# Reordering the start, the softmax exponentials and the last group's y in an attention, RWKV channel mix and gated convolution kernel

## The chip, the cores and the metric

One core of one Trainium2 chip. The metric is the device time of one execution in microseconds (us), the median of the runs. TensorE, VectorE, ScalarE, GpSimd and SyncE are PE, DVE, ACT, POOL and SP in the rows.

## What is computed

```python
w = np.exp(weight_gen - max); w = w / (sum(w) + 1e-9)       # softmax over 7 taps, 8 heads
x = causal 7-tap sum of x with weights w                      # attention, (2, 4160, 192)
xk, xr = mix of x and the token before it, with mu_k, mu_r
v = np.maximum(xk @ w_k, 0) ** 2 @ w_v                        # 192 -> 1024 -> 192
y = sigmoid(xr @ w_r) * v
h = np.maximum(y @ w_in, 0)                                   # 192 -> 1024
c = 3-tap convolution of h over the tokens, per channel
out = (h * sigmoid(c)) @ w_out                                # 1024 -> 192
```

## The kernel before

Each partition holds 65 consecutive tokens. They are worked through in 18 groups of 2, 2, 3, then fourteen times 4, and at last 2 token slots (a slot is 128 columns in the products); NG is the number of groups and NC = 8 the number of 128-wide chunks of the inner dimension. The order on each engine is written out by hand and kept by semaphores. In every group i the engines pass through two phases:

- `phase_a(i)`: PE makes the eight chunks of the first up product of group i+1 (`up1`, five matmuls each into one of the two PSUM banks `up0`, `up1`), the r product (`r_unit`), the transposes of y of group i (`yt_part`), and the down product of window i-1 (`down2`). ACT makes relu and square of each chunk (tile `ksq`), the high part of y, and the r sigmoid (tile `y`). DVE makes the low parts of y (`y_lo_part`), two convolution steps, the softmax of a later stretch of weights in two halves (`softmax_front`, `softmax_back`), and between the halves `attention(i+2)`.
- `phase_b(i)`: PE makes the second up product (`up2`), the down product of group i+1 (`down1`) and the transposes of attention (`t_part`). ACT makes the relu into `h` (`h_relu`), the first tap (`first_tap`), the gate's sigmoid (`gate_sigmoid`), and the copies `xt_copy` and `x_hi`. DVE makes the other taps and the gate (`window_step`), the mixes (`prep_k`, `prep_2`, `prep_r`), the low parts (`x_lo`), and y itself (`y_mult`).

A chunk of an up product may start when ACT has read the chunk two before it from the same bank. A `down1` or `down2` block is one token slot, eight matmuls of 128x192 (each stands as two in the trace).

`exps(n)` on ACT takes the exponential of stretch n of the attention weights. Exponential and sigmoid are in different activation tables; relu, square and copy need no load beside either. Stretch 0 is at the start, stretch 1 in `phase_b(0)`, stretches 2, 3 and 4 in `phase_a` of groups 2, 3 and 5.

At the very end the convolution wraps: the first two slots of `h` of group 0 are wanted again by the last window, so POOL copies them aside into `h3[:, :, KEEP + P:KEEP + 3 * P]`.

The start is a chain: the weights `wgt` arrive by three DMAs from ACT's queue, DVE makes the softmax of stretch 0, copies the parameters `prm` (which five DMAs bring, and PE transposes), then makes `attention(0)`, whose end lets PE start.

The end is written out too: `y_mult(NG - 1)`, `yt_part(NG - 1)`, `y_hi_part` and `y_lo_part` of the last group lie between the chunks of `up2(NG - 2)`, and `up2(NG - 1, 0)` needs what they make. The last group's parts use the tiles `xk_hi`, `xk_lo` and `xk2_s` (in rows `xk_s`).

Of the kernel before, what the change touches and what calls it, by code (L numbers as in the profile page):

```python
# [11 lines left out]
P = 128  # L12


def mixer_kernel(nc, x, weight_gen, mu_k, mu_r, w_k, w_v, w_r, w_in, conv_w, w_out, out):
# [58 lines left out]
    with ctx:  # L74
# [17 lines left out]
        prm = sb("prm", [P, NPRM])  # L92
        omu = sb("omu", [P, 3])

        wgt = sb("wgt", [P, (TPP + 1) * WROW])
# [56 lines left out]
        tap_act, tap, cv_ok, gs_ok, g_ok = [sem(n) for n in ("tap_act", "tap", "cv_ok", "gs_ok", "g_ok")]  # L152
        o_done, o_ok = sem("o_done"), sem("o_ok")
        h_keep, h_wrap, wrap_fix = [sem(n) for n in ("h_keep", "h_wrap", "wrap_fix")]
# [65 lines left out]
        def _(sp):  # L220
# [9 lines left out]

            S0 = size(0)
            sp.dma_start(xin[:, TAPS * D:(TAPS + S0) * D], x_rows[:, 0:S0 * D]).then_inc(x_in, 16)
            for a, b in HALO_RUNS:
# [38 lines left out]
        def _(pool):  # L272
# [20 lines left out]
            for g in range(3):  # L293
                double(g)

            pool.wait_ge(h_ok, NC)
            nc.gpsimd.tensor_copy(h3[:, :, KEEP + P:KEEP + 3 * P], h3[:, :, 0:2 * P]).then_inc(h_keep, 1)
            pool.wait_ge(h_keep, 1)
            double(3)
# [8 lines left out]
        def _(pe):  # L308
# [157 lines left out]
            for c in range(NC):  # L466
# [3 lines left out]
                if c == 5:  # L470
                    pe.wait_ge(wr_in, 32)
                    pe.wait_ge(wr_zero, 1)
                    r_unit(0, 0)
            pe.wait_ge(wv_in, 16)
            t_part(1, 1)
            t_part(1, 2)
            down1(0, 0)
            down1(0, 1)
# [17 lines left out]
            for c in range(NC):  # L496
                up2(NG - 2, c)
                if 1 <= c <= size(NG - 1):
                    down1(NG - 1, c - 1)
                if c == 4:  # L500
                    down2(NG - 3, 0)
                if c in (5, 6):
                    yt_part(NG - 1, c - 4)
                if c == 7:
                    down2(NG - 3, 1)
            for c in range(NC):
# [14 lines left out]
        def _(act):  # L521
# [52 lines left out]
            def h_relu(g, c):  # L574
                act.wait_ge(u2_done, NC * g + c + 1)
                if not eq(g, 0) and not eq(g, 1):
                    act.wait_ge(h_free, NC * n_windows(g - 1) + c + 1)
                at, n = h_home(g), size(g) * P
                nc.scalar.activation(h3[:, c, at:at + n], up[c % 2][:, 0:n], ACT.Relu).then_inc(h_ok, 1)  # L579

# [20 lines left out]
            def phase_a(i, with_y=True, with_out=True, with_o_copy=True, softmax_part=None, relus=0):  # L601

                for c in range(NC):
                    if c >= relus:
                        k_relu(i + 1, c)
                    if c >= 1:
                        k_square(i + 1, c - 1)
                    if with_y and c in (0, 2):
                        y_hi_part(i, c // 2 + 1)
                    if with_out and c in (0, 2):  # L610
                        gate_sigmoid(i - 1, EARLY + c // 2)
                    if c in (4, 6) and (c - 4) // 2 < len(units(i + 1)):
                        r_sigmoid(i + 1, (c - 4) // 2)
                k_square(i + 1, NC - 1)
                if softmax_part is not None:
                    exps(softmax_part)
                if with_out and with_o_copy:
                    for u in range(len(units(i - 1))):
                        o_copy(i - 1, u)

            def phase_b(i, with_t=True, with_win=True, softmax_part=None):
                for c in range(NC):
# [5 lines left out]
                    for part in t_parts_after(i, c) if with_t else ():  # L628
                        xt_copy(i + 2, part)
                    for part in t_parts_after(i, c - 2) if with_t else ():  # L630
                        x_hi(i + 2, part)
                    if c == 4 and softmax_part is not None:
                        exps(softmax_part)

# [5 lines left out]

            act.dma_start(wgt[:, WROW:SM_ENDS[1] * WROW], wg_rows[:, 0:(SM_ENDS[1] - 1) * WROW]).then_inc(wg_in, 16)
            for a, b in ((1, 16), (16, P)):
                act.dma_start(wgt[a:b, 0:WROW], before(wg_flat, a, b, 1, WROW)).then_inc(wg_in, 16)
            exps(0)
            act.wait_ge(wk_in, 48)
            nc.scalar.activation(wk_hi[:, :], raw_w(0), ACT.Copy).then_inc(w_cast, 1)
# [55 lines left out]
            for c in range(NC):  # L702
                h_relu(NG - 2, c)
                first_tap(NG - 2, c)
                if c >= 1:
                    gate_sigmoid(NG - 2, c - 1)
                if c in (6, 7):
                    y_hi_part(NG - 1, c - 5)
            gate_sigmoid(NG - 2, NC - 1)
# [23 lines left out]
        def _(dve):  # L733
# [247 lines left out]
            prep_r(2)  # L981
            x_lo(2, 1)
            y_mult(1, 0)
            x_lo(2, 2)
            softmax_back(1)
# [22 lines left out]
            for s in range(NC + 1):  # L1008
                window_step(NG - 2, s)
                if s == 3:  # L1010
                    y_mult(NG - 1, 0)
                if s in (6, 7):
                    y_lo_part(NG - 1, s - 5)
            for s in range(NC + 1):
                window_step(NG - 1, s)


            dve.wait_ge(h_free, NC * n_windows(NG))
            nc.vector.tensor_copy(h3[:, :, 2 * P:3 * P - 1], h3[:, :, KEEP + P + 1:KEEP + 2 * P]).then_inc(h_wrap, 1)
            nc.vector.tensor_copy(h3[:, :, KEEP + 1:KEEP + P], h3[:, :, P:2 * P - 1]).then_inc(h_wrap, 1)  # L1020
# [29 lines left out]
```

## Time and profile before

| | |
|---|---|
| time, median of 3 runs | 770.17 us (769.21 to 771.2) |
| profiled execution | 767.42 us, of which the span is 765.6 us |
| PE busy | 727.1 us, 95% of the span |
| DVE busy | 623.6 us, 81% |
| ACT busy | 485.5 us, 63% |
| POOL busy | 95.5 us, 12% |
| mean granted clock of PE | 0.995 of full speed |

The times on the left of the rows below are microseconds from the start of the span. The profiled execution was 2.75 us under the median of the other runs.

### The profile page before, as it was taken

The numbers are of one execution on the slowest core, as the hardware profiler recorded it, in microseconds if no ns is written. First come the engines' busy times: TensorE is split into PE (matmuls) and PEld (weight loads), VectorE is DVE, ScalarE is ACT, GpSimd is POOL, SyncE is SP. The second block draws the span as 40 slices with busy tenths as digits, with TensorE's granted clock in tenths as the row PEclk, the third lists the DMA queues.
The fourth block names the chain that finished last, engine by engine and source line by source line (L and its number), as shares of the span: only waits on it lengthen the run. The fifth ranks groups of instructions, "written<-read, shape, count | busy, mean of one in ns | idle before, by whom it ended". The sixth has DMA issues, their size and how long they took to land.

```text
span 765.6 us, 11918 instructions
## 1 busy us (share of the span) xinstructions
PE 727.1 (95%) x4043; PEld 664.8 (87%) x4043; DVE 623.6 (81%) x960; ACT 485.5 (63%) x913; POOL 95.5 (12%) x164
## 2 busy tenths in 40 slices
PE   0798989999999999999999999999999999999988
PEld 0697879998989899998989899898989999898988
DVE  5898899999699969869696988969696996937685
ACT  2557667676676747666674756667574765667764
POOL 1000101111110101101020111102010110101120
PEclk9999999999999999999999999999999999999999
DMA  7600110020202001020201002020200101000001
GB/s 180 212 2 0 52 63 1 0 68 1 73 1 73 0 25 49 0 72 0 72 0 61 11 0 72 0 72 0 72 0 12 60 0 62 1 22 0 1 9 55
DMA packets 8804, 27.82 MB, mean 36 GB/s; under 512 B 1007, under 2 KB 4041, under 8 KB 8647
## 3 DMA queue, kind: packets, MB, share of 16 engines
q1 hardware_dynamic: 8472, 27.21, 11.0%
q8 instruction: 17, 0.28, 0.1%
q10 hardware_dynamic: 302, 0.23, 0.1%
q14 instruction: 13, 0.10, 0.0%
HBM read 21.05 MB, written 6.39 MB: 36 GB/s over the span
## 4 chain that ended last, share of the span: by engine, by line
PE 87%; DVE 7%; ACT 4%; issue 1%; DMA 1%; ACTq 0%; DVEq 0%
PE up L346 37%; PE od L407 21%; PE dn L407 21%; PE mid L311 3%; PE dn L399 3%; PE dn L398 3%; DVE cv L855 1%; DVE prod L760 1%; DVE att L765 1%; DVE cv L857 1%; DMA wgt<-in_weight_gen 1%; ACT ksq L559 1%; ACT ksq L564 1%; DVE gat L865 1%; ACT L638 0%
## 5 line engine op out<-in xcount | busy, mean ns | idle before, releaser
L407 PE MATMUL dn<-wv_sb,ksq 128*128 128x192 f32 x1040 | 180.2, 327 | 0.7 <-ACT y L571 0.7
L407 PEld LDWEIGHTS dn<-wv_sb,ksq 128*128 128x128 f32 x1040 | 172.7, 191 | 5.7 <-ACT y L571 0.9
L855 DVE SCALAR_TENSOR_TENSOR cv<-h,prm,cv 128x512 f32<-128x512 f32 (+2 forms) x144 | 100.4, 697 | 89.5 <-ACT cv L586 88.8
L407 PE MATMUL od<-wo_sb,gat 128*128 128x192 f32 x944 | 160.9, 326 | 0.0
L407 PEld LDWEIGHTS od<-wo_sb,gat 128*128 128x128 f32 x944 | 155.3, 190 | 2.4
L559 ACT ACTIVATE ksq<-up 128x512 f32<-128x512 f32 (+2 forms) x144 | 80.0, 556 | 97.1 <-PE up L346 96.5
L291 POOL COPY h<-h 128x256 f32<-128x256 f32 x136 | 82.8, 609 | 428.0 <-DVE gat L865 396.6
L579 ACT ACTIVATE h<-up 128x512 f32<-128x512 f32 (+2 forms) x144 | 79.0, 550 | 88.9 <-PE up L346 88.8
L857 DVE SCALAR_TENSOR_TENSOR cv<-h,prm,cv 128x512 f32<-128x512 f32 (+2 forms) x144 | 101.2, 702 | 5.1
L586 ACT ACTIVATE cv<-h,prm 128x512 f32<-128x512 f32 (+2 forms) x144 | 97.9, 681 | 8.8 <-DVE h L1023 2.2
L765 DVE TENSOR_TENSOR att<-att,prod 128x768 f32<-128x768 f32 (+2 forms) x108 | 95.4, 883 | 1.6 <-DVE att L765 0.5
L760 DVE TENSOR_TENSOR prod<-xin,wgt 128x768 f32<-128x768 f32 (+2 forms) x108 | 96.0, 903 | 0.1
L591 ACT ACTIVATE cv<-cv 128x512 f32<-128x512 f32 (+2 forms) x144 | 83.6, 581 | 17.3 <-DVE cv L857 16.4
L865 DVE TENSOR_TENSOR gat<-h,cv 128x512 f32<-128x512 f32 (+2 forms) x128 | 82.3, 643 | 0.8
L564 ACT ACTIVATE ksq<-ksq 128x512 f32<-128x512 f32 (+2 forms) x144 | 82.9, 588 | 0.0
L346 PE MATMUL up<-xk_hi,wk_hi 128*128 128x512 f32 (+2 forms) x144 | 65.2, 452 | 4.2 <-ACT ksq L559 1.9
L346 PE MATMUL up<-y_hi,wi_hi 128*128 128x512 f32 (+2 forms) x136 | 63.5, 467 | 3.3 <-ACT h L579 3.2
L346 PE MATMUL up<-xk_hi,wk_lo 128*128 128x512 f32 (+2 forms) x144 | 54.7, 380 | 0.0
L346 PE MATMUL up<-xk_lo,wk_hi 128*128 128x512 f32 (+2 forms) x144 | 54.7, 380 | 0.0
L346 PE MATMUL up<-xk_s,wk_hi 128*128 128x512 f32 (+2 forms) x144 | 54.5, 378 | 0.2 <-DVE xk_s L828 0.2
L346 PE MATMUL up<-xk_s,wk_lo 128*128 128x512 f32 (+2 forms) x144 | 54.1, 376 | 0.0
L346 PE MATMUL up<-y_s,wi_hi 128*128 128x512 f32 (+2 forms) x136 | 51.7, 380 | 0.3 <-DVE y_s L848 0.3
(101 smaller groups left out, 978.5 us busy)
## 6 DMA issues: line engine op xcount, KB each, us to landing
xin<-in_x SPq DMA_DIRECT2D x13, 960.0 KB, 4.9
out<-o_sb SPq DMA_DIRECT2D x14, 384.0 KB, 2.3
wgt<-in_weight_gen SPq DMA_DIRECT2D x1, 1288.0 KB, 6.0
xin<-in_x SPq DMA_DIRECT2D x1, 864.0 KB, 4.7
wv_sb<-in_moe_w_v SPq DMA_DIRECT2D x1, 768.0 KB, 4.7
wo_sb<-in_moe_w_out SPq DMA_DIRECT2D x1, 768.0 KB, 7.8
xin<-in_x SPq DMA_DIRECT2D x1, 768.0 KB, 4.4
gat<-in_moe_w_k SPq DMA_DIRECT2D x1, 512.0 KB, 5.6
```

The costliest lines, as they stand in the source:

```text
L291: nc.gpsimd.tensor_copy(h3[:, c, 0:2 * P], h3[:, c, n:n + 2 * P]).then_inc(h_free, 1)
L346: mm = nc.tensor.matmul(dst[:, 0:n], w[:, cols], a[:, 0:n], start=(t == 0), stop=(t == len(terms) - 1))
L407: mm = nc.tensor.matmul(dst[:, n * D:(n + 1) * D], lhs(c)[:, b * P:(b + 1) * P], w[:, c, :], start=(c == 0), stop=(c == NC - 1))
L559: nc.scalar.activation(ksq3[:, c, 0:n], up[c % 2][:, 0:n], ACT.Relu).then_inc(k_ok, 1)
L564: nc.scalar.activation(ksq3[:, c, 0:n], ksq3[:, c, 0:n], ACT.Square).then_inc(ksq_ok, 1)
L586: nc.scalar.activation(conv_tile(w, c), win(w, c, 0), ACT.Copy, scale=prm[:, 3 + NC + c:4 + NC + c])\
L591: nc.scalar.activation(conv_tile(w, c), conv_tile(w, c), ACT.Sigmoid).then_inc(gs_ok, 1)
L760: nc.vector.tensor_tensor(v, x_tap(k), w_tap(k), ALU.mult)\
L765: nc.vector.tensor_tensor(acc, acc, term(k), ALU.add)\
L855: nc.vector.scalar_tensor_tensor(o, win(w, c, -1), taps[0], o, ALU.mult, ALU.add).then_inc(tap, 1)
L857: nc.vector.scalar_tensor_tensor(o, win(w, c, 1), taps[2], o, ALU.mult, ALU.add).then_inc(cv_ok, 1)
L865: nc.vector.tensor_tensor(gate_tile(w, c), win(w, c, 0), conv_tile(w, c), ALU.mult).then_inc(g_ok, 1)
```

## The change

It has six parts. (1) The main load of the first weights goes to SP's queue, ahead of x; ACT's queue keeps the two small ones, the larger of them first. (2) After the first exponential ACT makes a sigmoid of one column (tile `early`), and `down1(0, 0)` goes ahead of the transposes of group 1 on PE. (3) In `phase_b(0)` the exponential of stretch 1 moves from after the high parts of x to ahead of them, one chunk of `h` sooner, and the second x low part goes ahead of `y_mult(1, 0)` on DVE. (4) In `phase_a` the exponentials of stretches 2 to 4 move from behind the last square to behind the second r sigmoid, two squares and a relu sooner. (5) POOL's copy of the first slots of `h` goes; ACT writes each relu of group 0 twice instead, the kept one first. (6) The last group's `y_mult` is one step sooner on DVE, its transposes, high and low parts one chunk sooner, and two `down2` blocks of window NG - 3 later.

```diff
             S0 = size(0)
+            sp.dma_start(wgt[:, WROW:SM_ENDS[1] * WROW], wg_rows[:, 0:(SM_ENDS[1] - 1) * WROW]).then_inc(wg_in, 16)
             sp.dma_start(xin[:, TAPS * D:(TAPS + S0) * D], x_rows[:, 0:S0 * D]).then_inc(x_in, 16)
...
-            pool.wait_ge(h_ok, NC)
-            nc.gpsimd.tensor_copy(h3[:, :, KEEP + P:KEEP + 3 * P], h3[:, :, 0:2 * P]).then_inc(h_keep, 1)
-            pool.wait_ge(h_keep, 1)
             double(3)
...
             pe.wait_ge(wv_in, 16)
+            down1(0, 0)
             t_part(1, 1)
             t_part(1, 2)
-            down1(0, 0)
             down1(0, 1)
...
-                if c == 4:
-                    down2(NG - 3, 0)
-                if c in (5, 6):
-                    yt_part(NG - 1, c - 4)
-                if c == 7:
-                    down2(NG - 3, 1)
+                if c in (4, 5):
+                    yt_part(NG - 1, c - 3)
+                if c in (6, 7):
+                    down2(NG - 3, c - 6)
...
+                if eq(g, 0):
+
+                    nc.scalar.activation(h3[:, c, KEEP + P:KEEP + P + n], up[c % 2][:, 0:n], ACT.Relu)\
+                      .then_inc(h_keep, 1)
                 nc.scalar.activation(h3[:, c, at:at + n], up[c % 2][:, 0:n], ACT.Relu).then_inc(h_ok, 1)
...
                     if c in (4, 6) and (c - 4) // 2 < len(units(i + 1)):
                         r_sigmoid(i + 1, (c - 4) // 2)
+                    if c == 6 and softmax_part is not None:
+                        exps(softmax_part)
                 k_square(i + 1, NC - 1)
-                if softmax_part is not None:
-                    exps(softmax_part)
...
-                    for part in t_parts_after(i, c - 2) if with_t else ():
+                    if c == 3 and softmax_part is not None:
+                        exps(softmax_part)
+                    for part in t_parts_after(i, c - (1 if eq(i, 0) else 2)) if with_t else ():
                         x_hi(i + 2, part)
-                    if c == 4 and softmax_part is not None:
-                        exps(softmax_part)
...
-            act.dma_start(wgt[:, WROW:SM_ENDS[1] * WROW], wg_rows[:, 0:(SM_ENDS[1] - 1) * WROW]).then_inc(wg_in, 16)
-            for a, b in ((1, 16), (16, P)):
+            for a, b in ((16, P), (1, 16)):
                 act.dma_start(wgt[a:b, 0:WROW], before(wg_flat, a, b, 1, WROW)).then_inc(wg_in, 16)
             exps(0)
+
+            act.wait_ge(id_ok, 2)
+            nc.scalar.activation(early[:, :], ident[:, 0:1], ACT.Sigmoid).then_inc(early_ok, 1)
...
-                if c in (6, 7):
-                    y_hi_part(NG - 1, c - 5)
+                if c in (5, 6):
+                    y_hi_part(NG - 1, c - 4)
...
             x_lo(2, 1)
+            x_lo(2, 2)
             y_mult(1, 0)
-            x_lo(2, 2)
             softmax_back(1)
...
-                if s == 3:
+                if s == 2:
                     y_mult(NG - 1, 0)
-                if s in (6, 7):
-                    y_lo_part(NG - 1, s - 5)
+                if s in (5, 6):
+                    y_lo_part(NG - 1, s - 4)
...
+            dve.wait_ge(h_keep, NC)
```

On ACT in `phase_b(0)`, before, from the last squares of the phase ahead (`ksq`) through the relus (`h`), the x copies, the table load and exponential of stretch 1 (`wgt`):

```order
50 L564 ACTIVATE ksq<-ksq 128x256 x2
51 L579 ACTIVATE h<-up 128x256 x3
52 L528 ACTIVATE xt<-mid 128x384 x2
53 L579 ACTIVATE h<-up 128x256 x2
54 L536 ACTIVATE xk_hi<-xk 128x384
55 L539 ACTIVATE xk_s<-xkr 64x384
56 L638 ACT_TABLE_LOAD
57 L638 ACTIVATE wgt<-wgt 128x672
58 L579 ACTIVATE h<-up 128x256 x3
59 L559 ACTIVATE ksq<-up 128x384
```

The same place now, from the two x copies on; L577 is the kept relu and L579 the ordinary one:

```order
57 L524 ACTIVATE xt<-mid 128x384 x2
58 L577 ACTIVATE h<-up 128x256
59 L579 ACTIVATE h<-up 128x256
60 L638 ACT_TABLE_LOAD
61 L638 ACTIVATE wgt<-wgt 128x672
62 L532 ACTIVATE xk_hi<-xk 128x384
63 L535 ACTIVATE xk_s<-xkr 64x384
64 L577 ACTIVATE h<-up 128x256
65 L579 ACTIVATE h<-up 128x256
```

The exponential stands behind the fourth relu of the group instead of the fifth, ahead of both x high parts, and every relu is there twice.

On ACT in `phase_a(2)`, before, from the second r sigmoid (`y`) to the first relu of the next phase (`h`):

```order
123 L571 ACTIVATE y<-dn 128x384
124 L559 ACTIVATE ksq<-up 128x512
125 L564 ACTIVATE ksq<-ksq 128x512 x2
126 L638 ACT_TABLE_LOAD
127 L638 ACTIVATE wgt<-wgt 128x672
128 L598 ACTIVATE o_sb<-od 128x384
129 L579 ACTIVATE h<-up 128x384
```

The same place now:

```order
136 L567 ACTIVATE y<-dn 128x384
137 L638 ACT_TABLE_LOAD
138 L638 ACTIVATE wgt<-wgt 128x672
139 L555 ACTIVATE ksq<-up 128x512
140 L560 ACTIVATE ksq<-ksq 128x512 x2
141 L598 ACTIVATE o_sb<-od 128x384
142 L579 ACTIVATE h<-up 128x384
```

Table load and exponential went ahead of the last relu and the last two squares; nothing else moved.

On DVE near the end, before, from the gate of chunk 5 (into `xin`) of window NG - 2; `xk_lo` and `xk_s` are the last group's low parts of y:

```order
510 L865 TENSOR_TENSOR xin<-h,cv 128x512
511 L845 TENSOR_TENSOR xk_lo<-mid,xk_hi 128x256
512 L855 SCALAR_TENSOR_TENSOR cv<-h,prm,cv 128x512
513 L857 SCALAR_TENSOR_TENSOR cv<-h,prm,cv 128x512
514 L865 TENSOR_TENSOR prod<-h,cv 128x512
515 L848 TENSOR_TENSOR xk_s<-mid,xk_s 64x256
516 L865 TENSOR_TENSOR prod<-h,cv 128x512
```

The same place now, from the gate of chunk 4:

```order
507 L867 TENSOR_TENSOR xin<-h,cv 128x512
508 L847 TENSOR_TENSOR xk_lo<-mid,xk_hi 128x256
509 L857 SCALAR_TENSOR_TENSOR cv<-h,prm,cv 128x512
510 L859 SCALAR_TENSOR_TENSOR cv<-h,prm,cv 128x512
511 L867 TENSOR_TENSOR xin<-h,cv 128x512
512 L850 TENSOR_TENSOR xk_s<-mid,xk_s 64x256
513 L857 SCALAR_TENSOR_TENSOR cv<-h,prm,cv 128x512
514 L859 SCALAR_TENSOR_TENSOR cv<-h,prm,cv 128x512
515 L867 TENSOR_TENSOR prod<-h,cv 128x512 x2
```

Both low parts are one convolution step sooner; the last convolution (two rows into `cv`) now has both ahead of it, where it had one.

## Rows read from the trace of the kernel before

**Rows 1.** The page, shares of the chain that ended last.

```profile
PE 87%; DVE 7%; ACT 4%; issue 1%; DMA 1%; ACTq 0%; DVEq 0%
```

**Rows 2.** Who waited for whom, PE: us in total, times, longest.

```profile
PE mid L311 <- DVE att L765: 12.0, 2, 10.6
```

**Rows 3.** The chain in order of time, its first DMA: start, us, what.

```profile
1.92 4.93 DMA wgt<-in_weight_gen
```

**Rows 4.** Timeline of the first 13 us: start, us, engine, line; idle before and releaser.

```profile
4.18 0.30 SPq L239 DMA_DIRECT2D prm_rows<-in_moe_conv_w  x1
...
6.87 0.62 DVE L930 TENSOR_REDUCE smx<-wgt 128x64 f32<-128x448 f32 x1 [5.94 <-DMA wgt<-in_weight_gen]
...
9.53 0.27 PE L461 MATMUL mid<-ident,prm_rows 27*128 27x27 f32 x1 [9.53 <-DMA prm_rows<-in_moe_conv_w]
...
10.99 0.18 DVE L956 COPY prm<-mid 128x27 f32<-128x27 f32 x1
...
12.02 1.06 ACT L646 ACTIVATE wk_hi<-gat 128x1024 fp32r<-128x1024 f32 x1 [3.26 <-DMA gat<-in_moe_w_k]
```

**Rows 5.** Timeline around the first r sigmoid.

```profile
32.73 1.28 ACT L571 ACT_TABLE_LOAD   x1
...
34.57 5.47 PE L407 MATMUL dn<-wv_sb,ksq 128*128 128x192 f32 x32 [0.70 <-ACT y L571]
...
35.80 1.29 DVE L947 TENSOR_TENSOR wi_lo<-gat,wi_hi 128x512 fp32r<-128x512 f32 x2 [2.77 <-ACT wi_hi L659]
...
37.01 0.35 DVE L797 TENSOR_SCALAR xk<-xt,omu 128x256 f32<-128x256 f32 x1
```

**Rows 6.** Timeline of phase_b(0), and the exponentials by source line (ns min/median/max).

```profile
57.48 0.39 ACT L579 ACTIVATE h<-up 128x256 f32<-128x256 f32 x1 [2.81 <-PE up L346]
...
58.70 1.28 ACT L638 ACT_TABLE_LOAD   x1
...
61.09 0.39 PE L346 MATMUL up<-y_hi,wi_hi 128*128 128x256 f32 x1 [2.31 <-ACT h L579]
...
L638 ACT ACTIVATE wgt<-wgt x5: 576/768/1048, 8.2 to 238.3; 128x672 f32<-128x672 f32 x2, 128x448 f32<-128x448 f32 x1, 128x896 f32<-128x896 f32 x1, 128x1008 f32<-128x1008 f32 x1
```

**Rows 7.** Three windows: length, busy PE, PEld, DVE, ACT, POOL; granted clock, DMA, GB/s.

```profile
63.00:64.00 1.00, 1.00 (x6) 0.90 (x5) 1.00 (x1) 0.13 (x1) 1.00 (x1) 0.50 0.00 0
114.00:115.00 1.00, 1.00 (x5) 1.00 (x4) 0.96 (x3) 0.98 (x2) 0.00 (x0) 0.50 0.04 11
236.00:246.00 10.00, 10.00 (x59) 9.28 (x58) 9.20 (x12) 8.38 (x12) 0.40 (x1) 1.00 0.38 128
```

**Rows 8.** Timeline where phase_a(2) passes into phase_b(2).

```profile
111.49 0.66 PE L311 MATMUL mid<-ident,att 128*128 128x128 f32 x4 [1.39 <-DVE att L765]
...
112.84 0.69 PE L346 MATMUL up<-y_hi,wi_hi 128*128 128x384 f32 x1 [0.69 <-ACT h L579]
```

**Rows 9.** Timeline, y of group 3 and its transposes.

```profile
130.25 0.55 DVE L837 TENSOR_TENSOR y<-dn,y 128x384 f32<-128x384 f32 x1
...
131.74 0.60 PE L311 MATMUL mid<-ident,y 128*128 128x128 f32 x4
```

**Rows 10.** Timeline, the softmax after stretch 3 and y of group 4.

```profile
152.78 1.09 DVE L938 TENSOR_REDUCE smx<-wgt 128x128 f32<-128x896 f32 x1 [1.37 <-ACT wgt L638]
...
174.45 0.66 PE L311 MATMUL mid<-ident,y 128*128 128x128 f32 x4 [1.34 <-DVE y L837]
```

**Rows 11.** Timeline of the last group's y.

```profile
721.58 0.56 DVE L837 TENSOR_TENSOR y<-dn,y 128x384 f32<-128x384 f32 x1
...
730.47 0.63 ACT L591 ACTIVATE cv<-cv 128x512 f32<-128x512 f32 x1 [1.36 <-DVE cv L857]
...
731.07 0.43 DVE L848 TENSOR_TENSOR xk_s<-mid,xk_s 64x256 fp32r<-64x256 f32 x1
...
731.64 0.36 PE L346 MATMUL up<-xk_s,wi_hi 128*128 128x256 f32 x1 [2.23 <-DVE xk_s L848]
...
732.15 0.38 ACT L579 ACTIVATE h<-up 128x256 f32<-128x256 f32 x1 [1.05 <-PE up L346]
```

More of the change, by code:

```diff
@@ L93, in mixer_kernel @@
         omu = sb("omu", [P, 3])
+        early = sb("early", [P, 1])
         wgt = sb("wgt", [P, (TPP + 1) * WROW])
@@ L152, in mixer_kernel @@
         tap_act, tap, cv_ok, gs_ok, g_ok = [sem(n) for n in ("tap_act", "tap", "cv_ok", "gs_ok", "g_ok")]
-        o_done, o_ok = sem("o_done"), sem("o_ok")
+        o_done, o_ok, early_ok = sem("o_done"), sem("o_ok"), sem("early_ok")
         h_keep, h_wrap, wrap_fix = [sem(n) for n in ("h_keep", "h_wrap", "wrap_fix")]
```

## The prediction, made before the run

> **What bounds the kernel now.** I read the chain that ended last, then PE's waits, then the timelines where a wait stands. PE makes 87% of the chain [rows 1], so outside the first 20 us only time in which PE waits, or runs at its lower clock, can be won. The longest wait is the first, 10.6 us for attention(0) [rows 2]: the start is a chain of DMA, DVE and then PE. After it the waits are short and all where the hand-written order is special: before the first down product (0.70), in phase_b(0) (2.31), at the turn into phase_b(2) (1.39 and 0.69), at y of group 4 (1.34), at the last group's y (2.23) [rows 5, 6, 8, 10, 11]. Behind two of them the granted clock reads 0.50, that is 1.2 GHz instead of 2.4 [rows 7]. In the steady stretch between there is no wait to take away. The change touches each of these places.
>
> **Part 1, the weights first.** Now the last of three weight DMAs, the 112-partition one, is issued at 1.92 and takes 4.93 us [rows 3]; DVE starts at 6.87 and copies the parameters at 10.99, 4.12 us later, with no idle in between but that for the exponential [rows 4]. Afterwards that DMA is issued first on ACT's queue, some 1.1 us sooner, and the small one behind it; with the same 4.93 us the later of them lands at about 6.1, 0.75 sooner. The copy then could be at 10.2. But it also needs the parameters' transposes, which ran at 9.53 when the last of SP's five parameter DMAs, issued at 4.18, had landed [rows 4]. One more DMA ahead on SP's queue makes that issue about 0.4 us later; with the same 5.3 us to landing and 0.35 for the transpose the copy can be at 10.3. So 0.7 us is won, and DVE runs from there into PE's start without a wait. Bounds: nothing, if the big load delays the parameters by another 0.7; 1.1, if they land at 9.5 anyway and the weights sooner.
>
> **Part 2, the sigmoid's table.** The load of 1.28 us at 32.73 goes [rows 5]; the new one lies behind the first exponential, where ACT is idle for 3.26 us until w_k is there at 12.02 [rows 4]: 1.28 and a sigmoid of one column fit in. PE waits for that sigmoid, then makes 5.47 us of down product [rows 5]. With the table there the sigmoid ends at 33.2 instead of 34.5, and PE begins the first of the two blocks at once. But the next chain is DVE's: it waits for the cast of w_in on ACT until 35.80 (which can be 1.28 sooner), then splits for 1.2 us and mixes x of group 1 at 37.01 [rows 5]. That mix also needs the x copy, and its transposes now stand behind a down block of half of 5.47, 2.7 us: 33.25 + 2.6 to 2.7 + 0.3 for a transpose + 0.4 for the copy gives 36.55 to 36.7. So DVE wins only 0.3 to 0.46, not 1.28, and PE next needs what DVE makes. I take 0.4. Bounds 0 and 1.28. On this price the Trainium skill speaks too: its page ScalarE: Activation LUTs, section What ACT_TABLE_LOAD costs, counts about 1380 ns of drain besides 1283 ns of load, 2.66 us for a switch. The rows do not bear out the drain: from the load's start to PE's first matmul are 1.84 us, which hold the load and a sigmoid of 0.5, not 1.38 more. By the page the sum would still be the same 0.4, since DVE is what comes late.
>
> **Parts 3 and 5, the exponential in phase_b(0) and the kept slots.** ACT idles 2.81 us before the relu at 57.48, while PE makes a down block; at 58.70 table load and exponential begin, 1.28 + 0.77, and PE stands 2.31 us for the relu behind them [rows 6]. Moved ahead of the high parts, the 2.05 us fit into those 2.81. Not all is free: the two high parts (0.9 together) now lie between exponential and relu, and each relu of group 0 is made twice. I price a kept relu at 0.3 in a row of them, an estimate from the 0.39 of a single one [rows 6]; the eight are 2.4 us on ACT. Only those between two up products without a down block touch PE: one before the first down block (0.25), and those of the last chunks, where I get up1(2, 0) starting at 59.6 plus the earlier shift, against 62.0 now. The wait of 2.31 thus shrinks, net of 0.3 for the doubled relus, to a gain of 2.0. The half clock behind the wait goes with it: it held about 3.2 us [rows 7], in which work took twice as long, so 1.3 to 1.6 us. Sum 3.3. Bounds: 0.8 (each doubled relu in PE's way, 2.4, and part of the 0.9, against 2.31 + 1.6) and 3.9. POOL's copy of 1.9 us goes too; it ran beside DVE's last softmax step, and DVE begins attention(3) some 3.7 us sooner, as much as PE is ahead, so DVE does not become late. What would be next late is the sigmoid's table load for r of group 2, which both orders have.
>
> **Part 4, the exponentials in phase_a.** Three places, three answers. At group 2: PE's wait for attention, 1.39, stays, since DVE sets it; the 0.69 for the relu behind load and exponential goes [rows 8], as ACT makes them in the idle before the last relu. Behind these waits the clock was 0.50 for 3.2 us [rows 7], worth 1.6. If the clock stays up, PE is 2.3 ahead but DVE only 0.7; y of group 3 ends at 130.8 and PE took it at 131.74 [rows 9], a slack of 0.94, so of the 2.3 remain 0.7 + 0.94 = 1.6. If the clock drops all the same, 0.7. At group 3: DVE waits 1.37 for the exponential at 152.78, runs without idle to y of group 4, and PE waits there 1.34 [rows 10]; both go, 1.3. At group 5: DVE waits too, but PE is busy 10.00 of 10 us around it [rows 7], so 0.
>
> **Part 6, the last y.** PE waits 2.23 for xk_s at 731.64 [rows 11] and shortly before for xk_lo. With y_mult and the parts one chunk sooner xk_s is made around 728.5 and that wait goes. The next is ACT: the first relu of the last group (732.15) stands behind the last gate sigmoid, which waits for DVE's last convolution until 730.47. On DVE this convolution trades y_mult's 0.5, now in an idle place, for xk_s's 0.43 (0.56 and 0.43 in [rows 11]); so the sigmoid stays at 730.3, ends near 730.8, and the relu is at 730.8 instead of 732.15. PE needs that relu for its third chunk. Gain 1.3, bounds 0.5 and 2.7. The two down blocks moved behind have the gate's values long before.
>
> **The sum.** 0.7 + 0.4 + 3.3 + 1.6 + 1.3 + 0 + 1.3 = 8.6 us. From the profiled execution, 767.42 with a span of 765.6, that gives 758.8 and a span of 757.0. The median of the runs is 2.75 above the profiled one; I take the same difference off it: 770.17 - 8.6 = **761.6 us**.
>
> **The rivals.**
> - The clock. If the lower clock shows up behind a wait that stays (1.39 at group 2, or the new 1.5 near 729 while PE waits for the relu), 1 to 1.6 is lost once or twice: 762.6 to 764.8. For it: two stretches at 0.50 now [rows 7]. Against it: the wait of 2.23 at 731.64 had no slow matmuls behind it (0.36 us for the one shown) [rows 11], and the waits left are shorter. The Trainium skill, TensorE: Matmul & The Clock Gate, Part 1, says that the monitor runs freely, so that the point of change shifts from run to run; nothing here shows that yet.
> - The start gives nothing. The big load on SP's queue delays x or the parameters, which land together with much else; then 0.7 is lost and with an equal loss after it 762.3 to 763. For it: 5.3 us to landing already for 12 KB; against it: the bytes are the same, and all queues are drained together.
> - ACT becomes late in phase_b(0). Each doubled relu costs PE 0.3 and the high parts 0.9: parts 3 and 5 give 0.8 instead of 3.3, 764.1. Against it: the down blocks of 2.6 us lie between.
> - The preload does nothing, because the table is not kept until the r sigmoid. Then 762.0. Against it: relu, copy and square now follow sigmoids with no load.
> - Slower than before: the half clock in the steady stretch, brought by the new phase of the waits. Each us at 1.2 GHz costs half a us; from 17 us more of it the whole gain is gone; 30 us more give 776.6. For it nothing but the two stretches of 3.2 us; against it the mean granted clock in the busy stretches is 1.00 [rows 7].
>
> **Chances.** All parts as summed, 0.6; the clock lost once or twice, 0.17; ACT late, 0.08; the start without gain or the preload without effect, 0.1; so little that it is within 0.3% (2.3 us, about what a measurement of this kernel can tell from no change), 0.04; slower, 0.01. The range holds the sum's own doubt (0.7 at the start, 1 at the clock, 0.8 at the end), the clock rival and most of the one of ACT: 759.2 to 764.8. Faster by over 0.3%: 0.95; same 0.04; slower 0.01.
>
> **What would show it.** DVE's first reduction near 6.1 and the parameter copy near 10.2; the sigmoid near 32.5 with no load, PE's down block right behind it; the exponential of stretch 1 in the shadow of a down block and no clock of 0.50 near 62; PE's wait for attention(4) still 1.4, without the second; no wait at y of group 4; and at the end the wait for xk_s replaced by one of 1.5 us for the last group's first relu. I am wrong if ACT's relus hold PE in phase_b(0), if the parameters land over 0.7 later, or if the clock falls elsewhere.

## The result, and the profile after

The changed kernel takes **756.66 us** (median of 4 runs, 755.57 to 757.73), against 769.69 for the kernel before on the same chip (4 runs, 767.44 to 771.2). The ratio is 0.9833 with a 95% interval of 0.9804 to 0.9862: 13.0 us less, where 8.6 were forecast, and below the range. The profiled execution took 755.57 us, with a span of 753.8 against 765.6, so the two traces differ by 11.8 us, and it is those that are compared here.

The page of the kernel after, engines and chain (beside [rows 1]):

```profile
PE 722.0 (96%) x4043; PEld 661.9 (88%) x4043; DVE 621.4 (82%) x960; ACT 487.7 (65%) x922; POOL 94.0 (12%) x163
...
PE 85%; DVE 9%; ACT 3%; issue 2%; DMA 0%; SPq 0%; DVEq 0%; ACTq 0%
```

PE makes the chain as before. In order of time its first DMA is no longer the weights' of [rows 3] but that of the parameters (DMA 0% is the rounded share of its 3.50 us):

```profile
4.65 3.50 DMA prm_rows<-in_moe_conv_w
```

Who waited for whom (us in total, times, longest), beside [rows 2]:

```profile
PE mid L309 <- DVE att L767: 10.9, 2, 9.5
...
PE up L344 <- ACT h L579: 2.5, 6, 1.3
...
PE mid L309 <- DVE y L839: 0.7, 1, 0.7
```

The timeline of the first 20 us, for [rows 4]:

```profile
3.81 0.62 DVE L932 TENSOR_REDUCE smx<-wgt 128x64 f32<-128x448 f32 x1 [2.88 <-DMA wgt<-in_weight_gen]
...
5.71 1.28 ACT L646 ACT_TABLE_LOAD   x1
...
8.29 0.27 PE L459 MATMUL mid<-ident,prm_rows 27*128 27x27 f32 x1 [8.29 <-DMA prm_rows<-in_moe_conv_w]
...
8.60 0.18 DVE L958 COPY prm<-mid 128x27 f32<-128x27 f32 x1 [0.71 <-PE mid L459]
...
18.05 1.71 PE L309 MATMUL mid<-ident,att 128*128 128x128 f32 x6 [9.49 <-DVE att L767]
```

DVE starts 3.06 us sooner, not 0.75, and now waits for the parameters (0.71). The preloaded table lies at 5.71. For [rows 5], the timeline around the first r sigmoid:

```profile
30.16 0.48 ACT L567 ACTIVATE y<-dn 128x384 f32<-128x384 f32 x1
...
30.74 2.84 PE L405 MATMUL dn<-wv_sb,ksq 128*128 128x192 f32 x16 [1.21 <-issue]
...
31.92 1.29 DVE L949 TENSOR_TENSOR wi_lo<-gat,wi_hi 128x512 fp32r<-128x512 f32 x2 [1.28 <-ACT wi_hi L661]
...
34.25 0.35 DVE L799 TENSOR_SCALAR xk<-xt,omu 128x256 f32<-128x256 f32 x1 [1.03 <-ACT xt L524]
```

No table load stands there, PE's block follows the sigmoid at once, and DVE has a new wait of 1.03 us for the x copy. For [rows 6, 8, 9], one extract of the timeline each, phase_b(0), the turn into phase_b(2), and y of group 3:

```profile
52.46 1.28 ACT L638 ACT_TABLE_LOAD   x1
53.76 0.77 ACT L638 ACTIVATE wgt<-wgt 128x672 f32<-128x672 f32 x1
...
55.93 0.38 PE L344 MATMUL up<-y_hi,wi_hi 128*128 128x256 f32 x1 [0.39 <-ACT h L579]
...
105.82 0.66 PE L309 MATMUL mid<-ident,att 128*128 128x128 f32 x4 [1.40 <-DVE att L767]
106.23 0.42 PE L344 MATMUL up<-y_hi,wi_hi 128*128 128x384 f32 x1
...
124.39 0.66 PE L309 MATMUL mid<-ident,y 128*128 128x128 f32 x4 [0.67 <-DVE y L839]
```

The 2.31 of [rows 6] is 0.39 here, the 0.69 of [rows 8] is gone, the 1.39 has stayed, and a wait of 0.67 for y of group 3 is new. Two windows of the kernel after (columns as in [rows 7]) show the granted clock at 1.00, thus 2.4 GHz, where it read 0.50:

```profile
55.00:63.00 8.00, 7.45 (x48) 6.97 (x47) 7.80 (x12) 6.50 (x18) 0.00 (x0) 1.00 0.00 0
...
106.00:114.00 8.00, 8.00 (x52) 7.98 (x52) 7.75 (x14) 6.13 (x12) 0.81 (x2) 1.00 0.27 103
```

For [rows 11], the timeline where the last group begins. The relu stands behind the gate's last sigmoid, and PE waits for it:

```profile
719.80 0.63 ACT L591 ACTIVATE cv<-cv 128x512 f32<-128x512 f32 x1 [2.00 <-DVE cv L859]
720.34 0.36 ACT L579 ACTIVATE h<-up 128x256 f32<-128x256 f32 x1
720.76 0.39 PE L344 MATMUL up<-xk_hi,wi_hi 128*128 128x256 f32 x1 [1.35 <-ACT h L579]
```

The 11.8 us by stretch, from PE's landmarks in both traces (the transposes of attention and of y; the end of the steady stretch is the first up product behind the transposes of y of group NG - 2):

| stretch, up to | before | after | gained | forecast |
|---|---|---|---|---|
| first attention transpose | 20.44 | 18.05 | 2.39 | 0.7 |
| y of group 0 | 41.16 | 38.39 | 0.38 | 0.4 |
| attention of group 3 | 82.21 | 76.53 | 2.91 | 3.3 |
| attention of group 4 | 111.49 | 105.82 | -0.01 | 0 |
| y of group 3 | 131.74 | 124.39 | 1.68 | 1.6 |
| y of group 4 | 174.45 | 165.63 | 1.47 | 1.3 |
| end of the steady stretch | 700.34 | 690.04 | 1.48 | 0 |
| end | 765.6 | 753.8 | 1.50 | 1.3 |

Six of the eight are within 0.4 of the forecast. The start gave 1.7 more, and the steady stretch, to which nothing was ascribed, 1.5.

### The profile page after: what moved, and what is told of

Its sections match the earlier page's. It is cut to its first block, busy times and chain, and to the rows that moved or that the text cites. A ratio compares the mean times of both kernels' runs of the same rounds, so it can differ in the third digit from the quotient of the medians.

```text
span 753.8 us, 11926 instructions
## 1 busy us (share of the span) xinstructions
PE 722.0 (96%) x4043; PEld 661.9 (88%) x4043; DVE 621.4 (82%) x960; ACT 487.7 (65%) x922; POOL 94.0 (12%) x163
## 4 chain that ended last, share of the span: by engine, by line
PE 85%; DVE 9%; ACT 3%; issue 2%; DMA 0%; SPq 0%; DVEq 0%; ACTq 0%
PE up L344 35%; PE od L405 21%; PE dn L405 20%; PE mid L309 3%; PE dn L397 2%; PE dn L396 2%; DVE prod L762 2%; DVE att L767 1%; DVE cv L857 1%; DVE cv L859 1%; DVE gat L867 1%; ACT ksq L560 0%; DMA prm_rows<-in_moe_conv_w 0%; ACT h L579 0%; ACT ksq L555 0%
## 5 line engine op out<-in xcount | busy, mean ns | idle before, releaser
L579 ACT ACTIVATE h<-up 128x512 f32<-128x512 f32 (+2 forms) x144 | 79.1, 549 | 82.1 <-PE up L344 82.1
```

## The experiments

T below is the time of PE's first attention transpose. What lies behind it is measured as a distance between landmarks, so that a start that varies does not blur a later effect. Unless a diff says otherwise, an experiment is the kernel after with one edit.

**The start put back.** All three loads are issued as before: the big one (196 KB) on ACT's queue, then 15 rows, then 112.

```
-            sp.dma_start(wgt[:, WROW:SM_ENDS[1] * WROW], ...)
+            act.dma_start(wgt[:, WROW:SM_ENDS[1] * WROW], ...)
-            for a, b in ((16, P), (1, 16)):
+            for a, b in ((1, 16), (16, P)):
```

> The changed kernel with part 1 undone: all three weight loads on ACT's queue again, the big one first, then 15 rows, then 112 rows. Theory (the start was mis-sized): DVE's first reduction goes back from 3.81 to about 6.9 and PE's first attention transpose from 18.05 to 20.4; nothing behind it changes, so the span grows by 2.4 us to about 756.2. Rival (the 2.4 us of the start come from something else in that execution, such as a quicker memory): the first transpose stays near 18 and the span near 753.8.

**Only the order of the small loads put back** (the second of these edits alone).

> The changed kernel, big load on SP's queue, but on ACT's queue the 15 rows ahead of the 112 rows again. Theory (queue: what made the 112 rows slow before, 4.93 us to landing, was the big load ahead of them on the same queue): they still land in about 2.5 us, DVE's first reduction is at 3.8 to 4.6, and since DVE waits 0.7 us for the parameters anyway the first transpose stays at 18.05, the span at 753.8. Rival (order: they were slow because they were issued late, among the loads of x): reduction near 5.5 to 6, transpose near 19.5, span 755.2.

**Only the queue put back** (the first edit alone: big load, 112, 15, all on ACT's queue).

> The changed kernel with the big load first on ACT's queue, then 112 rows, then 15 rows; SP's queue as before the change. Theory (queue): the small loads are behind the big one and land near 6 as before; reduction at 6 to 6.9, first transpose at 19.6 to 20.4, span 755.3 to 756.2. Rival (order): the 112 rows are issued 0.4 to 0.7 us sooner than before and keep half of the gain, reduction near 5, transpose near 18.6 with the parameters as the limit.

| kernel | big load on | first reduction | parameter copy | T | time |
|---|---|---|---|---|---|
| after | SP | 3.81 | 8.60 | 18.05 | 755.57 |
| small loads in old order | SP | 4.02 | 10.27 | 19.72 | 758.1 |
| queue put back | ACT | 6.93 | 11.05 | 20.50 | 758.29 |
| all put back | ACT | 8.11 | 12.23 | 21.68 | 759.77 |

The queue decides. With the big load on SP's queue the order of the two small loads is worth 0.2. On ACT's it is 1.2 in this pair, but the kernel before, its repeat and its variant with an unused tile below have that same start and the reduction at 6.87 to 6.99, so the 8.11 belongs to that execution and not to the order. The DMA issues show it (KB each, median us from issue to landing), first those of the kernel after, then those with the queue put back:

```profile
wgt<-in_weight_gen SPq DMA_DIRECT2D x1, 196.0 KB, 2.7
...
wgt<-in_weight_gen ACTq DMA_DIRECT2D x1, 24.5 KB, 2.4
```

```profile
wgt<-in_weight_gen ACTq DMA_DIRECT2D x1, 196.0 KB, 3.8
...
wgt<-in_weight_gen ACTq DMA_DIRECT2D x1, 24.5 KB, 4.2
```

The same 24.5 KB take 4.2 us behind the big load on one queue, and 2.4 with the big load on the other (2.6 with them last in the old order). T is less tidy, since from there on the parameters decide. With the order put back the timeline has the weights at 4.02, yet

```profile
9.96 0.27 PE L459 MATMUL mid<-ident,prm_rows 27*128 27x27 f32 x1 [9.96 <-DMA prm_rows<-in_moe_conv_w]
10.27 0.19 DVE L958 COPY prm<-mid 128x27 f32<-128x27 f32 x1 [2.16 <-PE mid L459]
```

Over ten profiled executions with the start of the kernel after, the first reduction lies at 3.7 to 3.9, the copy at 8.6 to 10.3 and T at 18.05 to 19.74, 18.9 in the mean. With the big load on ACT's queue T was 20.44 to 20.55 in four executions, and 21.68 in one. So the start is worth 1.6 to 1.7 as a rule, and 2.4 in the execution that was profiled.

**Both kernels once more**, unedited, to see whether the pace of the steady stretch belongs to an execution or to the kernel.

> The kernel before, unchanged, for the steady stretch: PE took 43.83 us for a group of four slots before and 43.71 after, busy all the time in both, which makes 1.5 us over 12 groups. Theory (the pace belongs to the execution, not to the kernel): the groups of this execution take another time than 43.83, somewhere from 43.6 to 43.9. Rival (the change made each group shorter): again 43.83, and 43.71 in each of the three variants of the changed kernel. Also the half clock: if its place is free, the two stretches at 0.50 are not both near 61 and 113 again.

> The changed kernel as it is, for the comparison with the kernel named best on the same chip. Median 756 to 758. Its profile tells how far the start alone moves between executions: the parameters' copy somewhere from 8.6 to 10.3 and the first transpose from 18.05 to 19.7, with the same program.

The kernel before took 771.05 (span 769.2) and again needed 43.83 us for a group; the one after 757.03 (756.45 to 757.68), ratio 0.9831 (0.981 to 0.9852), its profiled T at 18.92. The pace is the kernel's. The half clock is not. In this execution the kernel before showed three stretches at 0.50, 13.7 us in all where the first had two and 6.8. One lies in phase_b(0), as before. One of 6.8 us begins within the 2.23 wait of [rows 11], where the first execution had none. The third begins at 35.5, behind PE's waits of 0.69 and 1.14 at the first down product, where the first had none either (1.14 and 0.70):

```profile
36.00:37.00 1.00, 1.00 (x5) 1.00 (x4) 0.64 (x2) 0.88 (x3) 0.00 (x0) 0.50 0.72 212
```

And at the turn into phase_b(2), with waits of 1.40 and 0.68 as in [rows 8], it had none.

**The place of the tiles.** The change adds a tile of one column, `early`, for the preloading sigmoid. It is allocated early and moves what follows by 32 bytes: xk_hi from 118496 to 118528 and y_hi from 144096 to 144128, from 32 beyond a multiple of 64 to a multiple of 64. Two experiments: the tile allocated last, so that these addresses are the old ones, and the kernel before with an unused tile of one column.

```
-        early = sb("early", [P, 1])        (kernel after: allocated last instead)
+        pad = sb("pad", [P, 1])            (kernel before: behind omu)
```

> The changed kernel with the one-column tile early made last instead of before wgt. Nothing is done otherwise; but all tiles from wgt on lie 32 bytes lower, so xk_hi, xk_lo, xk_s, y_hi, y_lo and y_s start at 32 beyond a multiple of 64 bytes as before the change, and not on a multiple of 64. Theory (place): PE's steady pace goes from 43.71 us per group of four slots back to 43.83 and a 512-column matmul from 231.5 to 233.1 ns, start to start; 1.5 us longer over the kernel. Rival (an instruction of the change made the pace): it stays 43.71.

> The kernel before with one unused tile of one column made behind omu and nothing else, so that all later tiles lie 32 bytes higher. Theory (place): PE's pace in the steady stretch goes from 43.83 to 43.71 us per group, 12 groups and some short ones, so 1.5 us less in all. Rival: it stays 43.83.

The timeline's transposes of y six groups apart, for before, before with the unused tile, after, and after with the tile last:

```profile
262.17 0.60 PE L311 MATMUL mid<-ident,y 128*128 128x128 f32 x4
...
525.17 0.60 PE L311 MATMUL mid<-ident,y 128*128 128x128 f32 x4
```

```profile
260.21 0.60 PE L312 MATMUL mid<-ident,y 128*128 128x128 f32 x4
...
522.45 0.60 PE L312 MATMUL mid<-ident,y 128*128 128x128 f32 x4
```

```profile
253.08 0.60 PE L309 MATMUL mid<-ident,y 128*128 128x128 f32 x4
...
515.32 0.60 PE L309 MATMUL mid<-ident,y 128*128 128x128 f32 x4
```

```profile
254.06 0.60 PE L309 MATMUL mid<-ident,y 128*128 128x128 f32 x4
...
517.08 0.60 PE L309 MATMUL mid<-ident,y 128*128 128x128 f32 x4
```

The distances are 263.00, 262.24, 262.24 and 263.02: 43.83 us a group with the operands at 32 beyond, 43.71 at multiples of 64, in either kernel. An unused tile makes the kernel before faster: 765.79 against 769.91 for it unchanged beside it. Of that the pace is 1.5; the rest goes with less half clock (one stretch in the profile, a mean granted clock of 0.997 against 0.993) and whether the tile has a part in that is not shown. The kernel after with the tile last took 757.83, with T at 18.51. Inside a chunk the 512-column up products start 1.6 ns sooner one after the other (means over ten groups of 232.2 and 233.8 ns), those that read xk's parts and those that read y's alike; some 80 of them in a group make the 0.13.

**The preload taken out** (the two lines of the wait and the sigmoid into `early`).

> The changed kernel without the early sigmoid (the tile stays, so nothing is placed otherwise); the 1.28 us table load is back in front of the first r sigmoid. Theory (DVE's chain is what comes late there): the lead gained between PE's first attention transpose and its transposes of y of group 0, 0.38 us with the change, goes and more, since the first down block now waits for the sigmoid and the x transposes stand behind it: 1.1 to 1.3 us lost against the changed kernel there. Rival (the preload is worth nothing, the down block's place is what counts): no loss at those transposes.

It took 760.56 (span 758.7), and from T to y of group 0 24.14 us instead of 20.3 to 21.2. The timeline and the window behind:

```profile
34.00 4.52 PE L405 MATMUL dn<-wv_sb,ksq 128*128 128x192 f32 x16 [2.63 <-issue]
...
39.19 0.35 DVE L796 TENSOR_SCALAR xk<-xt,omu 128x256 f32<-128x256 f32 x1 [2.72 <-ACT xt L524]
```

```profile
35.00:36.00 1.00, 1.00 (x5) 1.00 (x4) 0.82 (x2) 0.15 (x1) 0.00 (x0) 0.50 0.16 45
```

The load itself costs 1.4 of PE's wait (2.63 for 1.21). The block behind then runs at 0.50, takes 4.52 instead of 2.84, and the transposes of x, and with them DVE, come later by that too. In the kernel before the wait at this place was in two parts, with the transposes between them: 1.14 and 0.70 without a half clock behind in the first execution, 0.69 and 1.14 with one in the second.

**The exponential of stretch 1 put back** behind the high parts, a chunk later, and the high parts with it a chunk later too.

```
-                    if c == 3 and softmax_part is not None: exps(softmax_part)
-                    for part in t_parts_after(i, c - (1 if eq(i, 0) else 2)) ...: x_hi(i + 2, part)
+                    for part in t_parts_after(i, c - 2) ...: x_hi(i + 2, part)
+                    if c == 4 and softmax_part is not None: exps(softmax_part)
```

> The changed kernel with the exponential of stretch 1 back behind the x high parts, doubled relus kept. Theory (that exponential made the 2.31 us wait): PE waits 2.3 us or more in phase_b(0) again, for the relu, and starts the first up product of group 2 some 2.5 us later against PE's first transpose; if the clock falls behind it, up to 1.6 more. Rival (the wait was POOL's copy or the clock alone): under 1 us lost.

759.99 (span 758.2): the wait is back, with the half clock behind it, and from y of group 0 to attention of group 3 are 41.75 us instead of 38.14, 3.6 lost.

```profile
59.97 0.58 PE L344 MATMUL up<-y_hi,wi_hi 128*128 128x256 f32 x1 [2.58 <-ACT h L579]
```

```profile
61.00:62.00 1.00, 1.00 (x5) 1.00 (x5) 0.97 (x2) 0.56 (x2) 0.00 (x0) 0.50 0.00 0
```

**The kept slots given back to GpSimd** (POOL copies them, ACT makes each relu of group 0 once).

```
-                if eq(g, 0): nc.scalar.activation(h3[:, c, KEEP + P:KEEP + P + n], ...)
+            nc.gpsimd.tensor_copy(h3[:, :, KEEP + P:KEEP + 3 * P], h3[:, :, 0:2 * P])
```

> The changed kernel with part 5 undone: ACT makes each relu of group 0 once, POOL copies the first slots of h again. Theory (the doubled relus cost PE a little, POOL's copy costs DVE): PE reaches the first up product of group 2 up to 0.6 us sooner, and DVE's last step of the second softmax takes 2.5 us instead of 0.9, so that attention(3) starts 1.7 us later; PE behind it unchanged within 0.6 us. Rival (the copy held the chain): PE is over 1 us later at the transposes of attention of group 3.

756.64 (span 754.9), with T late at 19.74; from y of group 0 to attention of group 3 it needs 37.10 us, 1.04 less. The timeline shows the copy beside DVE's softmax step:

```profile
59.21 1.90 POOL L299 COPY h<-h 128x2048 f32<-128x2048 f32 x1 [7.37 <-ACT h L579]
...
60.10 1.71 DVE L943 TENSOR_TENSOR wgt<-wgt,smx 128x672 f32<-128x672 f32 x1
```

That step takes 1.71 instead of 0.86, but PE does not come to wait for it. This part of the change cost 1.0 and gave nothing.

**The exponentials of phase_a put back** behind the squares.

```
-                    if c == 6 and softmax_part is not None: exps(softmax_part)
                 k_square(i + 1, NC - 1)
+                if softmax_part is not None: exps(softmax_part)
```

> The changed kernel with part 4 undone: in phase_a the exponentials stand behind the last square again. Theory: PE waits 0.7 us again for the first relu at the turn into phase_b(2), loses 0.7 us there (1.6 to 2.3 if the clock falls there), waits 1.3 us at y of group 4 again, and loses nothing at group 5; 2.0 us in all, or about 3. Rival (only the softmax chain at group 3 counts): 1.3 us in all.

760.11 (span 758.3). From attention of group 3 to y of group 4 are 92.23 us instead of 89.10; of the 3.1, 1.74 are lost by y of group 3 and 1.4 at y of group 4.

```profile
107.28 0.66 PE L309 MATMUL mid<-ident,att 128*128 128x128 f32 x4 [1.40 <-DVE att L767]
...
108.60 0.44 PE L344 MATMUL up<-y_hi,wi_hi 128*128 128x384 f32 x1 [0.66 <-ACT h L579]
...
170.22 0.66 PE L309 MATMUL mid<-ident,y 128*128 128x128 f32 x4 [1.41 <-DVE y L839]
```

```profile
110.00:111.00 1.00, 1.00 (x4) 1.00 (x4) 1.00 (x2) 0.98 (x2) 0.00 (x0) 0.50 0.04 9
```

**The last y put back** by a chunk, with its transposes, high and low parts and down blocks.

```
-                if s == 2: y_mult(NG - 1, 0)
-                if s in (5, 6): y_lo_part(NG - 1, s - 4)
+                if s == 3: y_mult(NG - 1, 0)
+                if s in (6, 7): y_lo_part(NG - 1, s - 5)
```

> The changed kernel with part 6 undone: y_mult, transposes, high and low parts of the last group at their old places. Theory: PE waits 2.2 us for xk_s and 0.5 for xk_lo again and no longer 1.35 for the relu: 1.4 to 1.5 us longer, 755.2 for the span if the start is that of the changed kernel's profile. Rival (DVE's last gates bind, wherever the parts stand): under 0.5 us.

759.36 (span 757.6), with the end part 2.9 longer. The two old waits are back, and this time with a half clock:

```profile
719.57 0.39 PE L344 MATMUL up<-xk_lo,wi_hi 128*128 128x256 f32 x1 [0.54 <-DVE xk_lo L849]
...
722.18 0.36 PE L344 MATMUL up<-xk_s,wi_hi 128*128 128x256 f32 x1 [2.22 <-DVE xk_s L852]
```

```profile
723.00:724.00 1.00, 1.00 (x7) 1.00 (x7) 0.34 (x1) 0.82 (x3) 0.22 (x1) 0.50 0.00 0
```

**The relu ahead of the gate's last sigmoid.** If the 1.35 in the kernel after is the relu behind that sigmoid, moving it ahead removes it.

```
+            h_relu(NG - 1, 0)
             gate_sigmoid(NG - 2, NC - 1)
```

> The changed kernel with ACT's first relu of the last group ahead of the last gate sigmoid of the window before. Theory (the 1.35 us that PE waits there now are that order's): the wait goes, PE is 1.0 to 1.35 us sooner at the third chunk, and at most 0.3 us of it is lost behind, where the gate's sigmoid is later: end 0.7 to 1.3 us sooner. Rival (DVE is late as well, so the next relu waits for its convolutions): a new wait of nearly the same size on the fourth or fifth chunk, end within 0.3 us.

755.4 (span 753.6, T 18.50). The wait of 1.35 is gone, one of 0.64 for a later relu appears 4 us on, and from y of group NG - 2 to the end it is 0.7 shorter.

```profile
725.10 0.39 PE L344 MATMUL up<-xk_hi,wi_hi 128*128 128x256 f32 x1 [0.64 <-ACT h L579]
```

**The parameters on ACT's queue** (the five loads issued by ACT behind the small weight loads, instead of by SP behind the big one).

> The changed kernel with the five small parameter loads on ACT's queue behind its two weight loads, not on SP's behind x. Theory (with the weights in by 3.8 us the parameters set the start: the copy of prm was at 8.6 to 10.3 in nine executions while the softmax was done near 7.9): the transposes of the parameters run near 6, the copy follows the softmax at 7.9 to 8.0, unless the activation table, now loaded later, holds the first exponential up; PE's first attention transpose at 17.3 to 17.6 instead of 18.05 to 19.7. Rival (x lands with the parameters and is next): the copy is early but attention(0) waits, and the transpose stays at 18 to 19.

755.81 (span 754.0), T 17.92, 0.9 sooner than the mean, but not the 17.3 to 17.6 of the theory. The copy stands at 7.93 without a wait, and the next in line is x, as the rival had it:

```profile
8.89 0.76 DVE L762 TENSOR_TENSOR att<-xin,wgt 128x576 f32<-128x576 f32 x1 [0.57 <-DMA xin<-in_x]
```

**The down block behind the transposes of x** (the order of the kernel before; the preload stays).

```
-            down1(0, 0)
             t_part(1, 1)
             t_part(1, 2)
+            down1(0, 0)
```

> The changed kernel with the first down block behind the x transposes of group 1 again, sigmoid table still early. Theory (the block ahead of them holds DVE 1.03 us, since DVE's mix waits for the x copies): DVE runs from the w_in split into the mix without that wait and PE, which needs the low parts of x, is about 1.0 us sooner at the transposes of y of group 0 (19.3 to 20.2 after its first transpose instead of 20.3 to 21.2, and 0.2 to 0.5 less if the down blocks themselves come late). Rival (PE's down blocks are what binds): no gain or 0.3 us lost, since PE idles before the transposes.

756.24 (span 754.5), T 19.17. The wait of 1.03 is gone; the mix follows the split at once:

```profile
33.76 1.29 DVE L949 TENSOR_TENSOR wi_lo<-gat,wi_hi 128x512 fp32r<-128x512 f32 x2 [1.99 <-ACT wi_hi L661]
34.97 0.35 DVE L799 TENSOR_SCALAR xk<-xt,omu 128x256 f32<-128x256 f32 x1
```

From that split's start to y of group 0 are 5.34 us here, 6.47 in both executions of the kernel after: the moved block cost 1.1. From T it is 19.93 instead of 20.34 and 20.86, since what lies between T and the split varies by some 0.7 between executions.

**All four together**: parameters on ACT's queue, down block behind, kept slots on GpSimd, relu ahead.

> The changed kernel with four things together: parameter loads on ACT's queue, the down block behind the x transposes, POOL's copy of the first slots of h instead of ACT's doubled relus, and the last group's first relu ahead of the last gate sigmoid. If the theories hold they add: 1.0 (doubled relus, as measured by undoing them) + 0.7 (relu ahead, as measured) + 0.5 to 1.5 (parameters) + 0.5 to 1.0 (down block) = 2.7 to 4.2 us under the changed kernel, about 753 us. Rival (they cover each other: what is won before the first relus is lost at the next wait of DVE): 1.5 to 2 us.

**752.50 us** (752.36 to 752.61, 4 runs), ratio to before 0.9772 (0.9752 to 0.9792), 4.5 under the 757.03 of the kernel after. That is more than the 2.7 to 4.2 of the theory. T is 17.33, 1.6 sooner than in the profile of the kernel after beside it (18.92), and the next stretches are 19.72 and 37.09 instead of 20.3 to 20.9 and 38.1 to 38.2; so the four add up and do not cover each other.

## Why the prediction was wrong in size and right in kind

- **Part 1** (0.7, bounds 0 and 1.1): the mechanism was DVE starting sooner; the size was not. The first step that failed is "with the same 4.93 us". That landing time was taken as a property of the small load, but it was what the load had ahead of it on its queue. With the big load elsewhere it is 2.4, and the reduction starts 3.06 sooner, not 0.75. The text saw rightly that the parameters limit the rest. Here their transposes ran 3.6 us after the last issue (8.29, issued at 4.65) and not the 5.3 that [rows 4] gave; in another execution they were late enough for the copy to stand at 10.27, as forecast. The term was 1.6 to 1.7 as a rule, 2.4 in the profiled one.
- **Part 2** (0.4) measured 0.38. The reason given is right: DVE is what comes late, and the block ahead of the transposes eats most of the 1.28; without that block 1.1 comes back. That the size is hit so closely is luck: the same stretch took 20.3 to 21.2 us between executions that have the same order there, and 20.72 and 21.47 in the kernel before and in it with the unused tile. What the text did not see is that the load alone, with the new order, would have brought a half clock: the two edits are worth 3.3 against an order that has only the second.
- **Parts 3 and 5** (3.3) measured 2.91. The wait and the half clock went as summed; the 0.3 set for the doubled relus was 1.04, and so the copy on POOL would better have stayed.
- **Part 4** (0, 1.6 and 1.3) measured -0.01, 1.68 and 1.47: the wait for attention stayed at 1.40 by the profile, y of group 3 capped the gain with a wait of 0.67, and y of group 4 has no wait.
- **Part 6** (1.3) measured 1.50, and the wait that was named as the next one, for the last group's first relu, is there with 1.35, against the 1.5 forecast. Put ahead of the sigmoid it gives 0.7 and hands over to the next relu.
- **The missing term.** The sum had "in the steady stretch between there is no wait to take away", which is true, and took from it that nothing changes there, which is not. The new tile moves the operands by 32 bytes, and each 512-column up product is 0.7% faster: 1.5 us. This is the second step that failed: the account of the change names the tile, and the prediction put the effect of its place at nothing without a reason. The weights' tiles did not move, and the products that read xk's parts and those that read y's both gained; what in the matmul reads slower from such an address stays open.
- **The conversion to the median.** The same 2.75 between profiled execution and median was carried over. It is 1.1 for the kernel after (756.66 - 755.57), 2.3 for the one before (769.69 - 767.42). The second execution of before had 6.8 us more at half clock, which is 3.4 of the 3.6 by which its span is longer; after the change neither profile of the kernel shows any while PE works, so there is less to vary. That this is all of the difference between 2.3 and 1.1 is argued, not shown.
- **The rivals.** The clock did not fall behind the waits that stayed. But how near it was is shown by the four experiments that restore one wait of 2.2 to 2.6 us, or in one case 1.40 and 0.66 in a row: each had exactly one stretch at 0.50 while PE worked, right behind. The 2.23 of the first execution of before had none, that of the second had one; the 2.31 of phase_b(0) had one in both, but none in the kernel before with the unused tile. The Trainium skill, TensorE: Matmul & The Clock Gate, Part 1, says that the point of change shifts from run to run; here even whether the change comes differs between executions of one program. The rival of the start did not come, ACT late in phase_b(0) came with 0.7 of its 2.5, the preload held, and the steady stretch lost no clock.

By terms, the forecast of 8.6 lacked 1.7 at the start and 1.5 in the pace and had 0.4 too much in phase_b(0); the other terms are 0.4 short in sum: 8.6 + 1.7 + 1.5 - 0.4 + 0.4 = 11.8.

## What to carry to other kernels

A transfer's time from issue to landing is what its queue had ahead of it as much as its own size; before keeping it in a sum, ask what is left ahead of it, and what is waited for next when it comes sooner. A short wait of PE is worth more than its length where the granted clock falls behind it, so price the two together, and expect the second half in some executions only. Look at what a new tile does to the addresses behind it: in a kernel in which PE is busy all the time, 32 bytes were worth as much as a moved exponential.

## What the runs showed of the hardware

- fp32r matmuls of 512 columns start 232.2 ns apart in the mean with the moving operands (the parts of xk and y) at multiples of 64 bytes, and 233.8 ns with them 32 bytes beyond, in both kernels.
- A load of 24.5 KB landed 2.4 to 2.6 us after its issue, and 4.2 to 6.2 with a 196 KB load ahead of it on the same queue; the parameter loads' landing varied by 1.7 us between executions of one start.
- A tensor-tensor operation of 672 columns on DVE took 0.86 us, and 1.71 when it began while POOL's copy ran. In the second execution of the kernel before it began 0.2 us ahead of the copy: there it took 0.86, and the copy 2.40 instead of 1.90.
- The granted clock fell within or right behind seven of nine single waits of PE of 2.2 to 2.6 us, and behind two of four pairs of about 1.4 and 0.7 and one of two of 1.1 and 0.7; behind none of the waits of 1.2 to 1.5 us that are alone. It is not the same in every execution of one program.
